# Linear attention with a dense tail: four-tile products mixed between products of head pairs

## What is computed

```python
def _attn_ref(q, k, v, beta):
    B, H, S, D = q.shape                      # 4, 8, 768, 48
    k_n = k / (norm(k, axis=-1) + 1e-06)
    state = zeros((B, H, D, D)); y = zeros_like(q)
    for t in range(S):
        kt, vt, bt = k_n[:, :, t], v[:, :, t], beta[:, :, t, None]
        y[:, :, t] = einsum('bhd,bhde->bhe', q[:, :, t], state)
        v_old = einsum('bhde,bhd->bhe', state, kt)
        state = state + bt[..., None] * einsum('bhd,bhe->bhde', kt, vt - v_old)
    return y
```

## Time and profile before

| | us |
|---|---|
| median of 3 executions | 844.03 |
| all three | 843.44, 844.03, 848.15 |
| the profiled execution, its own time | 849.1 |
| its span, first to last instruction | 847.3 |
| PE busy | 787.1 (93%) |
| DVE busy | 512.8 (61%) |
| ACT busy | 318.5 (38%) |
| POOL busy | 164.8 (19%) |

### The profile page before, as it was taken

How to read it: one execution, slowest core, us unless ns; L and a number is a source line. 1 busy time by engine, 2 the same in 40 slices (tenths; PEclk the granted TensorE clock), 3 DMA queues, 4 the chain that set the end, 5 groups by cost and what they waited for, 6 DMA issues and landing times.

```text
span 847.3 us, 24876 instructions
## 1 busy us (share of the span) xinstructions
PE 787.1 (93%) x10976; PEld 554.7 (65%) x10976; DVE 512.8 (61%) x1238; ACT 318.5 (38%) x635; POOL 164.8 (19%) x201
## 2 busy tenths in 40 slices
PE   4688888898889999999999999999999999999998
PEld 3688788888878556565655566655666666666664
DVE  4997777777747675633473336455545767758522
ACT  3465555565442251212221224232333443533211
POOL 2542323232200001300130000002132323323100
PEclk9999999999998799999999999999999999999999
DMA  8133533332121131010001000000000000000101
GB/s 205 32 85 79 142 79 79 79 78 60 41 79 40 56 112 56 1 57 0 29 29 56 1 29 29 1 1 1 1 1 1 2 29 20 29 10 29 38 19 56
DMA packets 44813, 37.54 MB, mean 44 GB/s; under 512 B 27360, under 2 KB 38818, under 8 KB 44706
## 3 DMA queue, kind: packets, MB, share of 16 engines
q1 hardware_dynamic: 37925, 30.90, 12.8%
q10 hardware_dynamic: 6781, 5.05, 2.4%
HBM read 26.50 MB, written 4.72 MB: 37 GB/s over the span
## 4 chain that ended last, share of the span: by engine, by line
PE 78%; DVE 10%; issue 5%; ACT 4%; DMA 2%; SPq 0%; ACTq 0%; POOL 0%; DVEq 0%
PE bank L305 14%; PE bank L1081 6%; PE bank L1083 6%; PE bank L1129 6%; PE bank L1127 6%; PE bank L1128 6%; PE bank L1082 6%; PE bank L1065 3%; PE bank L1067 3%; PE bank L1066 3%; PE bank L337 3%; DVE hT_lo L1520 2%; PE bank L1000 2%; PE bank L1004 2%; PE bank L360 1%
## 5 line engine op out<-in xcount | busy, mean ns | idle before, releaser
L1245 ACT ACTIVATE hT_hi<-bank 128x384 f16<-128x384 f32 x96 | 46.8, 489 | 161.3 <-PE bank L1067 161.2
L1520 DVE SCALAR_TENSOR_TENSOR hT_lo<-bank,hT_hi 128x384 f16<-128x384 f32 x96 | 53.2, 555 | 71.2 <-ACT hT_hi L1245 71.0
L1065 PE MATMUL bank<-unT,wA 128*128 128x384 f16 x288 | 94.0, 326 | 2.0 <-DVE unT L1514 1.3
L1081 PE MATMUL bank<-wA,hT_hi 128*128 128x384 f16 x288 | 94.0, 326 | 1.4 <-DVE hT_lo L1520 1.4
L1067 PE MATMUL bank<-unT,wA 128*128 128x384 f16 x288 | 93.9, 326 | 0.0
L1066 PE MATMUL bank<-unT,wA 128*128 128x384 f16 x288 | 93.9, 326 | 0.0
L1083 PE MATMUL bank<-wA,hT_lo 128*128 128x384 f16 x288 | 93.9, 326 | 0.0
L1082 PE MATMUL bank<-wA,hT_hi 128*128 128x384 f16 x288 | 93.9, 326 | 0.0
L305 PE MATMUL bank<-Yv,ET 64*64 64x48 f32 x2304 | 75.6, 219 | 5.5 <-issue 2.9
L305 PEld LDWEIGHTS bank<-Yv,ET 64*64 64x64 f32 x2304 | 73.5, 136 | 8.0 <-ACT Yv L443 4.4
L443 ACT ACTIVATE Yv<-bank,rows 128x384 f32<-128x384 f32 x72 | 40.5, 577 | 70.6 <-PE bank L305 70.4
(11 more groups left out here) (212 smaller groups left out, 1684.1 us busy)
## 6 DMA issues: line engine op xcount, KB each, us to landing
Kb<-k_dram SPq DMA_DIRECT2D x24, 192.0 KB, 3.6
Vv<-v_dram SPq DMA_DIRECT2D x12, 384.0 KB, 3.9
z_first<-w_dram SPq DMA_DIRECT2D x8, 576.0 KB, 4.2
z_first<-wt_dram SPq DMA_DIRECT2D x8, 576.0 KB, 3.6
out_dram<-hT_hi SPq DMA_DIRECT2D x24, 192.0 KB, 1.9
KQ<-q_dram SPq DMA_DIRECT2D x44, 96.0 KB, 2.4
X<-Yo ACTq DMA_DIRECT2D x12, 192.0 KB
X<-Yo ACTq DMA_DIRECT2D x10, 189.0 KB
```

Of the source, the lines that this page charges most:

```text
L1065: pe.matmul(out, w1[0][:, k, cols], unT[0][:, k, :], start=(k == 0), stop=False)
L1081: pe.matmul(out, hT[0][:, f, cols], w2[0][:, f, :], start=(f == 0), stop=False)
L1245: act.activation(hT[0][:, f, :], bank[3 + m % 3][:, 0:TG * P], ACT.Relu).then_inc(s_hh, 1)
L1520: dve.scalar_tensor_tensor(hT[1][:, f, :], bank[3 + m % 3][:, 0:TG * P], 0.0, hT[0][:, f, :], ALU.max, ALU.subtract).then_inc(s_hl, 1)
```

## The change

Only the attention's TensorE list and the head of DVE's list change. The four-tile products that were blocks of their own are cut into steps and issued between pairs:

- `predicted` goes between the first four pairs of corner 1 (two steps behind each). It stood ahead of corner 0.
- The gram halves go between the last pairs of solve's and hop 1's second half, the last step behind the half.
- `hop(c, 3)` and `queried` become `last_hop`: two steps of queried between its halves, six between the pairs of its second half.
- `grow` goes between the first four pairs of direct 1. It stood ahead of direct 0.
- DVE makes `mask_e(c, 0)` ahead of `make_x(c)`.

No product, copy or load is added or taken away, and ACT, POOL and SP keep their lists.

```diff
             def corner(n, u):
                 if not there(n):
                     return
-                pe.wait_ge(s_ab, 4 * n + 4)
-                pe.wait_ge(s_tt, 2 * n + 2)
+                if u == 0:
+                    pe.wait_ge(s_ab, 4 * n + 4)
+                    pe.wait_ge(s_tt, 2 * n + 2)
                 out = take("E", n, u)
                 for j in range(HG):
                     g = u * HG + j
                     mm = pair(out[:, j * C:(j + 1) * C], Ab[:, n % RA, g], TT[:, g], True, True)
+                    if u == 1 and n >= 1 and j < HG // 2:
+                        predicted_step(n, 2 * j)
+                        predicted_step(n, 2 * j + 1)
                 mm.then_inc(s_e, 1)
...
             def solve(c):
...
                     pe.wait_ge(s_xe, 2 * c + a + 1)
+                    beside = a == 1 and there(c + 2)
                     for j in range(HG):
                         g = a * HG + j
                         mm = pair(chain(a)[:, j * D:(j + 1) * D], TT[:, g], Yv[:, c % 2, g], j == 0, True)
+                        if beside and j == 3:
+                            out = gram_banks(c + 2, (0, 2))
+                        if beside and 3 < j < HG - 1:
+                            gram_step(c + 2, (0, 2), j - 4, out)
                     mm.then_inc(s_Y, 1)
+                    if beside:
+                        gram_step(c + 2, (0, 2), HG // 2 - 1, out)
...
+            def last_hop(c):
...
+                for a in range(2):
+                    pe.wait_ge((s_ya, s_yd)[a], 4 * c + 3)
+                    for j in range(HG):
+                        g = a * HG + j
+                        mm = pair(chain(a)[:, j * D:(j + 1) * D], ET[:, g], Yv[:, c % 2, g], False, True)
+                        if c and a == 1 and j < HG - 2:
+                            queried_step(c, j + 2, out)
+                    mm.then_inc(s_Y, 1)
+                    if a == 0:
+                        out = [take("O", c, u)[:, 0:HG * D].rearrange("p (g d) -> p g d", g=HG) for u in range(2)]
+                        if c:
+                            queried_step(c, 0, out)
+                            queried_step(c, 1, out)
                 return out
...
             def direct(c, a, out):
...
                 for j in range(HG):
                     g = a * HG + j
                     mm = pair(out[a][:, j], PT[:, c % RA, g], Yv[:, c % 2, g], c == 0 and j == 0, True)
+                    if a == 1 and c < LAST and j < HG // 2:
+                        grow_step(c, 2 * j)
+                        grow_step(c, 2 * j + 1)
                 mm.then_inc(s_O, 1)
...
             for c in range(C0, NC):
-                predicted(c)
                 corner(c, 0)
                 corner(c, 1)
                 solve(c)
-                gram(c + 2, (0, 2))
+                if c < 0:
+                    gram(c + 2, (0, 2))
                 hop(c, 1)
-                gram(c + 2, (1, 3))
+                if c < 0:
+                    gram(c + 2, (1, 3))
                 hop(c, 2)
                 turn(c + 3)
-                hop(c, 3)
-                out = queried(c)
-                grow(c)
+                out = last_hop(c)
                 direct(c, 0, out)
                 direct(c, 1, out)
...
             for c in range(C0, NC):
+                mask_e(c, 0)
                 make_x(c)
-                mask_e(c, 0)
                 mask_e(c, 1)
```

More of the change, by code:

```diff
@@ L326, in turn, with gram_banks, gram_step, gram @@
                     mm.then_inc(s_T, 1)
-            def gram(n, parts):
-                if not there(n):
-                    return
+            def gram_banks(n, parts):
                 pe.wait_ge(s_kt, 2 * n + 2)
                 pe.wait_ge(s_qd[n % RT], 64 * (n // RT + 1))
[L333 to L339, removed]
+                return [take("GP", n, u) for u in parts]
+            def gram_step(n, parts, j, out):
+                m = parts[0] * HG // 2 + j
+                for h, r in TILES:
+                    mm = pe.matmul(out[r][half[h], j * P:(j + 1) * P], KQ[feat[r], n % RT, 0, h, m],
+                                   KQ[feat[r], n % RT, :, h, m], start=True, stop=True, skip_group_check=True)
+                if j == HG // 2 - 1:
+                    mm.then_inc(s_gp, 1)
+            def gram(n, parts):
+                if there(n):
+                    out = gram_banks(n, parts)
+                    for j in range(HG // 2):
+                        gram_step(n, parts, j, out)
+            def predicted_step(c, m):
+                if m == 0:
+                    pe.wait_ge(s_ya, 4 * c)
+                    pe.wait_ge(s_yd, 4 * c)
+                    pe.wait_ge(s_se, 2 * c)
+                for h, r in TILES:
+                    mm = pe.matmul(chain(r)[half[h], m * D:(m + 1) * D], KQ[feat[r], c % RT, 0, h, m],
+                                   Sv[feat[r], c % 2, h * HG + m], start=m == 0, stop=True, skip_group_check=True)
+                if m == HG - 1:
+                    mm.then_inc(s_X, 1)
             def corner(n, u):
@@ L381, in hop @@
                         pe.wait_ge(s_et, 2 * c + a + 1)
+                    beside = k == 1 and a == 1 and there(c + 2)
                     for j in range(HG):
@@ L384, in hop @@
                         mm = pair(chain(a)[:, j * D:(j + 1) * D], ET[:, g], Yv[:, c % 2, g], False, True)
+                        if beside and j == 3:
+                            out = gram_banks(c + 2, (1, 3))
+                        if beside and 3 < j < HG - 1:
+                            gram_step(c + 2, (1, 3), j - 4, out)
                     mm.then_inc(s_Y, 1)
-            def queried(c):
+                    if beside:
+                        gram_step(c + 2, (1, 3), HG // 2 - 1, out)
@@ L388, in queried, with queried_step @@
+            def queried_step(c, m, out):
+                for h, r in TILES:
+                    mm = pe.matmul(out[r][half[h], m], KQ[feat[r], c % RT, 1, h, m], Sv[feat[r], c % 2, h * HG + m],
+                                   start=m == 0, stop=False, skip_group_check=True)
+                if m == HG - 1:
+                    mm.then_inc(s_oq, 1)
+            def last_hop(c):
                 if c < 0:
                     return None
-                out = [take("O", c, a)[:, 0:HG * D].rearrange("p (g d) -> p g d", g=HG) for a in range(2)]
@@ L391, in queried @@
[L391 to L396, removed]
-                return out
+                for a in range(2):
[11 more added lines that the diff above has]
+                            queried_step(c, 1, out)
@@ L399, in direct, with grow_step @@
+                return out
+            def grow_step(c, m):
+                for h, r in TILES:
+                    mm = pe.matmul(state(h)[feat[r], m * D:(m + 1) * D], key(c, h, r, m), Yv[half[h], c % 2, r * HG + m],
+                                   start=c == 0 and m == 0, stop=True, skip_group_check=True)
+                if m == HG - 1:
+                    mm.then_inc(s_S, 1)
             def direct(c, a, out):
@@ L401, in direct @@
                     return
-                pe.wait_ge(s_pt, 4 * c + 4)
+                if a == 0:
+                    pe.wait_ge(s_pt, 4 * c + 4)
+                    if c:
+                        pe.wait_ge(s_oq, c)
+                    else:
+                        pe.wait_ge(s_zs, 2)
                 pe.wait_ge((s_ya, s_yd)[a], 4 * c + 4)
-                if c:
-                    pe.wait_ge(s_oq, c)
                 for j in range(HG):
```

## The result

The changed kernel takes a median of 856.66 us (852.08 to 860.38, 4 executions) against 843.74 us (840.89 to 848.15, 4 executions) before: a ratio of 1.0156, 95% interval 1.0117 to 1.0196. That is 12.9 us slower; forecast were 8.4 us and 852.4, with a range of 842 to 864. A later comparison of the same two kernels gave 1.0100 (1.0065 to 1.0135).

The account below looks back on a forecast made before the run. TensorE was taken to bound the kernel, with code-fetch stalls in the attention. New waits of 20.9 + 5.5 + 2.5 less 20.5 us of stalls gave +8.4 us, from 844.0 to 852.4 us, range 842 to 864.

Parts of the forecast that it names:

- What bounds the attention: Attention: TensorE sets the time; 27.1 us of issue stalls come from code arriving at about 256 instructions per 3.5 us.
- No gain in array time: Mixed stretches: diagonal quarters still take pair and four-tile records in turn, 58 + 56 ns as in blocks; gain 0.
- Wait 1: Corner: PE newly waits for ACT's TT, made after grow's state copies; 1.9 us in 11 chunks, 20.9 us.
- the prediction's own signs: Profile after: no TT wait named means Wait 1 wrong; faster mixed stretches mean B; issue above 15 us means rival C.
- rival C: TensorE's list: code stalls stay, or alternating costs PE at each seam; up to +28.9 us, 872.9 us; chance 0.13.
- Wait 2: Solve: PE newly waits for X from DVE, which corner used to cover; 0.5 us, 11 times, 5.5 us.
- Wait 3: ACT's chain of gram copies, Dy, Yv ending in hop 3: AP copies start 0.25 us later, ten chunks, 2.5 us.
- What is given back: Attention: mixed order consumes code more evenly, so 20.5 of 27.1 us of issue stalls go and 6.6 remain.
- A: Attention: the waits leave fetching ahead and all 27.1 us of stalls go; +1.8 us, 845.8 us, no change; chance 0.19.
- B: Mixed stretches: quarters fill each other's gaps, up to 4.2 us of block time a stage; -30 us, 814 us; chance 0.13.

Follow-up runs that it names:

- The two fillers: Kernel before plus, behind direct 1, 14 identity transposes (28 records of code): 851.99 us; or 14 identity pairs (112 records), nearly equal array time: 863.21 us.
- the parts mixed alone: Kernel before with one product mixed, the others in blocks: queried 850.44 us, gram 847.51, grow 850.25, predicted (TT made ahead of the state copies) 848.79.
- TT first: Changed kernel with ACT making TT of the next chunk ahead of the state copies, mixed order kept: 850.86 us, ratio 1.0030.

## Why the prediction was right, and where it was off

- **What bounds the attention: right.** Stalls "issue" follow the code. The two fillers show it without the mix, and the stalls stand 256 records apart or a multiple of it. The prediction's 252 records a packet left out the 268 semaphore instructions in the list; with them it is 255.
- **No gain in array time: right.** 0.23 to 0.24 us for a pair and a step, against 0.228 worked out from blocks. The stages at full clock even have 0.5 us more busy time.
- **Wait 1: right, a little too large.** 1.8 us in nine of eleven chunks (1.9 forecast), 17.8 us in all for 20.9. In the other two a code stall in direct, just ahead, took half of its place. The prediction expected the profile to name ACT's TT; it wrote "issue". By the prediction's own signs (no wait for TT named, issue above 15 us) wait 1 would have been wrong and rival C right. The place and the end of TT settle it; those signs relied on a name that the profile infers.
- **Wait 2: right in place, too large.** 0.39 us where it shows, and 2.0 us in all for 5.5; in half of the chunks other delays came first. Some 0.9 us more in chunk 0, where the mask now stands ahead of X's copies, were not in the sum.
- **Wait 3:** PE's wait for ACT's Yv ahead of the hops is 4.3 us for 2.6, which is 1.7 of the 2.5 forecast. Grow's own 0.7 of before has gone, so 1.0 is left.
- **What is given back: right.** Issue waits other than those for TT are 5.8 us up to 274 us, and 7.7 to the end of the attention, as a stall of 1.9 at 274.16 follows. 6.6 had been forecast to remain of 27.1.
- **The term that was missing: the clock.** The new waits measured are 17.8 + 2.0 + 0.9 + 1.0 = 21.7 us, and 27.1 - 7.7 = 19.4 were given back. That leaves +2.3, in line with the 2.7 us more that PE idles over the span, and less than the +8.4 forecast. The other 8.6 us of this execution are busy time, and it ran at low clock. The sum and the profile thus agree in their terms and not in their balance, which is a small difference of large ones: that 8.4 came so near 12.9 is partly luck.
- **How much the clock is worth stays open.** Over many executions it differs less: the kernel before had a mean of 0.989 over 27, the changed one 0.984 over five, and the stages at full clock and the two executions at like clock still show a loss of about 1 us a stage and of some 8 us. In the first comparison the changed kernel had 0.968, 0.975, 0.994 and 0.975; of the kernel before only the profiled execution's clock is known there, 0.985. A lower clock may be why the loss was 12.9 us there and 10.3 in the second, but that is not shown. No profile shows the changed kernel at the clock of the kernel before.
- **Rivals.** A (stalls go whole, no change) fell because the waits are as large as what they pay for. B, and C in the size that it was given, fell with the parts mixed alone.

No version here beats the kernel before. With TT first, the changed kernel and the version with predicted as a block come within 0.3 to 0.4% of it. The order changes neither the number of instructions nor the time that they take to arrive, but each of these two still has a wait that the blocks had covered (for X in one, for Sv in the other), so whether a mix without any could win is open.

## What to carry to other kernels

Where TensorE issues small products, count instructions as well as array time: here stalls 256 records apart were at least 3.3 us apart, and reordering does not make the list shorter. To tell such a stall from a wait, look at its number in the list: it keeps its place in the count of 256 when the order changes, and a wait does not. Before cutting a block up to fill idle quarters, ask which quarter is the fullest, and which copies on other engines the block was covering: grow's and predicted's places decided when TT and X were waited for. A new wait that lies where a stall lay costs only the difference, so undo one part at a time before adding up. And each block put back brought its own wait with it: grow waited for Y, predicted for Sv.

## What was not expected

- The granted clock went with the order: 0.97 before and 0.92 with the waits, over 36 to 270 us of the profiled executions, 0.96 with TT first, and 0.99 when the longest wait was filled with products. In the first 36 us it differed between runs (0.77 to 1.00) without such a reason.
- A higher clock was not worth time in this stage: with code as the next limit, 859.6 us at 0.990 on average are no better than 858.4 at 0.984.
- Some 17 us of extra array time in the kernel before cost 5.5 us, as long as they came in few instructions.
